# Gated attention and two FFNs on one core: the last two blocks of the first FFN in groups of 15 block products

## The reference

```python
# attention: 4 x 8 heads, 768 steps, head size 48; f = sigmoid(f_logit)
for t in range(S):
    state = f[:, :, t, :, None] * state + np.einsum('bhd,bhe->bhde', k[:, :, t], v[:, :, t])
    y[:, :, t] = np.einsum('bhd,bhde->bhe', q[:, :, t], state)
# x: 3072 tokens x 384
x = ((x @ w_a) * (x @ w_b)) @ w_out            # first FFN, 1536 hidden
p = domain_probs / (domain_probs.sum(-1, keepdims=True) + 1e-09)
for e in range(4):                             # second FFN, 4 x 1024 hidden
    h = np.maximum(x @ w1[e], 0.0)
    out += p[:, e:e + 1] * (h @ w2[e])
```

## Time and profile before

| | us |
|---|---|
| median of 3 runs | 1306.95 (1306.39 to 1307.71) |
| the profiled execution | 1305.98 |
| its span, first to last instruction | 1304.2 |
| PE busy | 1297.3 (99%) |
| DVE busy | 847.8 (65%) |
| ACT busy | 621.1 (48%) |
| POOL busy | 548.4 (42%) |

### The profile page before, as it was taken

How to read it: one execution, slowest core, us unless ns; L and a number is a source line. 1 busy time by engine, 2 the same in 40 slices (tenths; PEclk the granted TensorE clock), 3 DMA queues, 4 the chain that set the end, 5 groups by cost and what they waited for, 6 DMA issues and landing times.

```text
span 1304.2 us, 25769 instructions
## 1 busy us (share of the span) xinstructions
PE 1297.3 (99%) x9391; PEld 1269.5 (97%) x9391; DVE 847.8 (65%) x1668; ACT 621.1 (48%) x1259; POOL 548.4 (42%) x560
## 2 busy tenths in 40 slices
PE   9999999999999999999999999999999999999998
PEld 8999999999999999999999999999999999999998
DVE  8866565566533324277777777777677776777765
ACT  7654444444332323355445554445544545545442
POOL 3331211222136764324445644446544447444441
PEclk9999999999999999999999999999999999999999
DMA  8512122122204343123222343222342323343211
GB/s 262 166 43 68 47 63 67 49 61 67 57 16 132 101 143 120 50 79 97 91 86 80 91 134 89 95 82 69 108 133 88 98 64 95 96 130 98 88 59 49
DMA packets 71695, 117.74 MB, mean 90 GB/s; under 512 B 7120, under 2 KB 49808, under 8 KB 71568
## 3 DMA queue, kind: packets, MB, share of 16 engines
q1 hardware_dynamic: 71568, 116.08, 29.4%
HBM read 102.94 MB, written 14.55 MB: 90 GB/s over the span
## 4 chain that ended last, share of the span: by engine, by line
PE 98%; DVE 1%; DMA 0%; POOL 0%; issue 0%; ACT 0%; SPq 0%; DVEq 0%; POOLq 0%
PE bank L1964 12%; PE bank L1966 11%; PE bank L1965 11%; PE bank L2198 11%; PE bank L2199 10%; PE bank L2200 10%; PE bank L2094 5%; PE bank L2092 5%; PE bank L2093 5%; PE score_banks L2092 3%; PE score_banks L2094 3%; PE score_banks L2093 3%; PE bank L1954 2%; PE bank L1958 2%; PE score_banks L1883 1%; PE score_banks L1912 1%
## 5 line engine op out<-in xcount | busy, mean ns | idle before, releaser
L1291 POOL TENSOR_TENSOR wu<-w_r,wu 128x640 fp32r<-128x640 f32 (+1 forms) x132 | 200.6, 1522 | 314.8 <-ACT wu L976 314.8
L2198 PE MATMUL bank<-wd,h_hi 128*128 128x384 f32 x768 | 259.9, 338 | 0.3 <-issue 0.3
L2199 PE MATMUL bank<-wd,h_hi 128*128 128x384 f32 x768 | 257.6, 335 | 0.0
L2200 PE MATMUL bank<-wd,h_lo 128*128 128x384 f32 x768 | 257.1, 335 | 0.0
L1733 DVE SCALAR_TENSOR_TENSOR xt<-bank,pn,xt 128x384 f32<-128x384 f32 x288 | 177.1, 615 | 100.5 <-PE bank L2200 91.2
L1003 ACT ACTIVATE h_hi<-h 128x384 fp32r<-128x384 f32 x240 | 124.6, 523 | 192.9 <-DVE h L1683 81.1
L1964 PE MATMUL bank<-xs_hi,wab 128*128 128x384 f32 x570 | 196.7, 345 | 0.4 <-ACT a_sb L1014 0.4
L1965 PE MATMUL bank<-xs_hi,wab 128*128 128x384 f32 x570 | 191.0, 335 | 0.0
L1966 PE MATMUL bank<-xs_lo,wab 128*128 128x384 f32 x570 | 190.9, 335 | 0.0
L1296 POOL TENSOR_TENSOR wd<-raw,wd 128x384 fp32r<-128x384 f32 x128 | 133.4, 1056 | 87.6 <-ACT wd L981 83.6
L1704 DVE SCALAR_TENSOR_TENSOR h_lo<-h,h_hi 128x384 fp32r<-128x384 f32 x240 | 135.6, 579 | 50.1 <-ACT h_hi L1003 45.0
(11 more groups left out here) (203 smaller groups left out, 2668.1 us busy)
## 6 DMA issues: line engine op xcount, KB each, us to landing
w_r<-weight_sums SPq DMA_DIRECT2D x120, 320.0 KB, 2.9
raw<-w SPq DMA_DIRECT2D x48, 576.0 KB, 3.9
unit<-fkq SPq DMA_DIRECT2D x28, 504.0 KB, 4.5
v_in<-v_chunks SPq DMA_DIRECT2D x32, 144.0 KB, 4.1
out<-xt SPq DMA_DIRECT2D x24, 192.0 KB, 4.4
weight_sums<-w_s SPq DMA_DIRECT2D x10, 384.0 KB, 4.5
weight_sums<-w SPq DMA_DIRECT2D x40, 64.0 KB, 2.8
raw<-w SPq DMA_DIRECT2D x6, 384.0 KB, 3.2
```

Of the source, the lines that this page charges most:

```text
L1291: eng.tensor_tensor(wu_piece(g, n, 1), wu_raw(g, n), wu_piece(g, n, 0).bitcast(f32), ALU.subtract).then_inc(s_ulo, 1)
L2198: eng.matmul(o, hh, w_hi, start=(f == fs[0]), stop=False)
L2199: eng.matmul(o, hh, w_lo, start=False, stop=False)
L2200: mm = eng.matmul(o, hl, w_hi, start=False, stop=(f == fs[-1]))
```

## The change

Only 6 blocks of the first FFN run in the plain way (`PLAIN` = 6, `N1` = 72 hidden tiles). The last two blocks become a pass of groups of 15 products like those of the second FFN. `PASSES` lists one pass of the first FFN and four of the second, `GROUPS` all of their groups. The pass has 8 groups of three hidden tiles each, alternately for a (`makes_a`, into `h2`) and for b (`makes_h`, into `hb`). POOL multiplies the two (`product`, 6 operations per pair of groups), ACT rounds (`h1_round`), DVE makes the rest (`h1_rest`), and PE applies the down weights for a pair of groups in the next two groups (`down`), with DVE adding the tiles (`weigh`).

```diff
+    PLAIN = 6
+    N1 = PLAIN * FT1
+    PASSES = [(1, b) for b in range(PLAIN // 2, NP)] + [(2, b) for b in range(NP)]
+    GROUPS = [(p, q) for p, (ffn, _) in enumerate(PASSES) for q in (range(2 * NF) if ffn == 1 else (NQ, *range(NQ)))]
+    NS = 2 * NF + NQ
...
-    SUMS_AT, SUMS_PACE = CMIN_AT, 8
+    SUMS_AT, SUMS_PACE = 31, 9
```

```diff
                 if n == 0:
                     eng.wait_ge(s_wr, w_loads(q))
-                    eng.wait_ge(s_wst[q % 2], W_STORED * (q // 2)) if q >= 2 else eng.wait_ge(s_y, NU)
+                    if q:
+                        sums_stored(eng, q - 1)
...
+            def product(g, n):
+                o = H_ORDER[n]
+                eng.wait_ge(s_add, adds(g) + (3, 6, 7, 8, 9, 10)[n])
+                eng.tensor_tensor(hb[:, o, :], h2[:, o, :], hb[:, o, :], ALU.mult).then_inc(s_mul, 1)
```

The running sum of a unit was one scan of 384 elements, with a buffer of factors that reset it, and a minimum; it becomes six scans of 64:

```diff
-                if u >= FIRST:
-                    c = unit_ring[ring(u)][0:P2, F, :]
-                    eng.tensor_tensor_scan(c, reset[0:P2, :], c, 0.0, ALU.mult, ALU.add).then_inc(s_scan, 1)
-                    eng.wait_ge(s_scan, u - FIRST + 1)
-                    eng.tensor_scalar(c, c, CMAX, None, ALU.min).then_inc(s_cum, 1)
-                    return
-                for cc in range(CPU):
-                    c = unit_ring[ring(u)][0:P2, F, cc * CH:(cc + 1) * CH]
-                    eng.tensor_tensor_scan(c, c, cmax[0:P2, :], 0.0, ALU.add, ALU.min).then_inc(s_cum, 1)
+                n = CH if u < FIRST else HC
+                for cc in range(UT // n):
+                    c = unit_ring[ring(u)][0:P2, F, cc * n:(cc + 1) * n]
+                    eng.tensor_tensor_scan(c, c, cmax[0:P2, 0:n], 0.0, ALU.add, ALU.min).then_inc(s_cum, 1)
```

Operations of DVE on two tensors in SBUF become `scalar_tensor_tensor` with a factor of 1; those that read PSUM (`gate`, `add`) stay:

```diff
+            def two_inputs(to, a, b, op):
+                return eng.scalar_tensor_tensor(out=to, in0=a, scalar=1.0, in1=b, op0=ALU.mult, op1=op)
...
-                eng.tensor_tensor(h_lo[:, i % 2, 0:TB1], h_sb[:, :], h_hi[:, i % 2, 0:TB1].bitcast(f32),
+                two_inputs(h_lo[:, i % 2, 0:TB1], h_sb[:, :], h_hi[:, i % 2, 0:TB1].bitcast(f32),
                                   ALU.subtract).then_inc(s_hlo, 1)
```

On PE the down tiles of the first FFN stand in other places than those of the second:

```diff
+                    elif ffn(g) == 2:
+                        down(g - 1, n)
+                    elif makes_a(g):
+                        if n == 2:
+                            down(g - 1, 0)
+                        elif n == 5:
+                            down(g - 1, 1)
+                    elif q_of(g) > 1:
+                        if n == 0:
+                            down(g - 2, 2)
+                        elif n == 3:
+                            down(g - 2, 3)
+                        elif n == 5:
+                            down(g - 2, 4)
+                            down(g - 2, 5)
```

More of the change, by code:

```diff
@@ L356, in gated_attention_then_two_ffns @@
         s_wcp = sem("s_wcp")
[L357 removed]
+        s_wst = sem("s_wst")
         s_wu = [sem(f"s_wu{n}") for n in range(3)]
@@ L508, in f_tiles, with makes_a, makes_h, full @@
+        def makes_a(g):
+            return ffn(g) == 1 and q_of(g) % 2 == 0
+        def makes_h(g):
+            return not makes_a(g)
+        def full(g):
+            return ffn(g) == 1 or q_of(g) < NQ
+        def sums_of(g):
+            return q_of(g) if ffn(g) == 1 else 2 * NF + q_of(g)
         def f_tiles(q):
             return range(FG * q, FG * q + (FG if q < NQ else LAST))
-        def shares(g):
-            fs = f_tiles(g % GP)
+        def fs_of(g):
+            return range(FG) if ffn(g) == 1 else range(len(f_tiles(q_of(g))))
@@ L526, in results, with products, parts @@
+        def products(g):
+            return sum(2 * FG if ffn(x) == 1 and makes_h(x) else 0 for x in range(g))
         def results(g):
-            return sum(2 * len(f_tiles(x % GP)) for x in range(g))
+            return sum(2 * len(fs_of(x)) for x in range(g) if makes_h(x))
+        def parts(g):
+            return len(shares(q_of(g))) if ffn(g) == 2 else 1
         def tiles(g):
-            return sum(TT * len(shares(x)) for x in range(g))
+            return sum(TT * parts(x) for x in range(g) if makes_h(x))
@@ L1079, in _ @@
                     split_hi(HI_AT[j])
-                for n in range(1, NB1):
+                for n in range(1, PLAIN):
                     for k in range(KT):
@@ L1101, in _ @@
                     copy(g, 0)
                     copy(g, 1)
-                    if g:
-                        up_round(g + 1, 0)
-                    if change:
-                        x2_round(change, 0)
-                        x2_round(change, 1)
+                    for n in range(FG):
+                        down_round(g, n)
+                    plain_hi(nxt, 2)
+                    for n in range(3):
+                        sum_hi(nxt, n)
+                    copy(g, 2)
+                    plain_hi(nxt, 3)
@@ L1108, in _ @@
+                    up_round(g + 2, 0)
+                    h2_round(g, 4)
+                    up_round(g + 2, 1)
+                    h2_round(g, 5)
+                    up_round(g + 2, 2)
+                    down_round(g + 1, 0)
+                elif full(g):
+                    copy(g, 0)
+                    copy(g, 1)
+                    for n in range(FG):
+                        down_round(g, n)
                     copy(g, 2)
                     h2_round(g, 0)
-                    if g:
-                        up_round(g + 1, 1)
@@ L1318, in _ @@
                             x1_lo(n, k)
-                for q in range(NQ):
+                for q in range(NS):
                     for n in range(16):
```

810 lines of the change are left out of this document (517 added, 293 removed).

## The result

The changed kernel takes 1413.4 us (median of 4 runs, 1408.3 to 1418.4), the kernel before 1307.1 (1306.4 to 1307.7): a ratio of 1.081 with a 95% interval of 1.080 to 1.083. The prediction had 1301.3 us and faster: sign and size are wrong. The profiled execution took 1408.3, its span is 1406.5 us.

What follows compares the result with a forecast made beforehand. It took PE, busy 99% of the span, as the bound. 1305.98 - 12.5 + 0.7 + 0.2 + 3.2 + 1.3 + 1.5 = 1300.4, with the runs' median 0.97 higher: 1301.3 us, range 1296.5 to 1308.

Steps and rivals of the forecast that it cites:

- every rival: Full gain 1294 to 1298, 0.16; attention 1305 to 1309, 0.17; POOL's sums 1312, 0.08; POOL with DVE 1312, 0.05.
- 72 matmuls less, 12.5 us: First FFN's last two blocks: four pairs of groups save 72 matmuls at 0.1738 us each, 12.5 us less.
- The scalar costs 0: DVE's operations on two SBUF tensors: `scalar_tensor_tensor` takes as long as `tensor_tensor`, 0 with 2 ns each way.
- a budget: Pair of groups in the new pass: POOL 19.1, DVE 17.9 and ACT 12.7 us, none reaching PE's 25.0.
- a pass above 183 us: Sign of being wrong: a pass of the second FFN takes more than 732 / 4 = 183 us.
- POOL and DVE together, the last rival: New pass: from 2.3 us more blocking a pair they pass PE's 25.0; at 5 us, 1312; chance 0.05.
- Groups 0 to 2, 1.25 + 0.25 + 1.0 + 1.2: New pass's start: PE waits before products 4 and 13 of group 1, then products 2 and 4 of group 2.
- the -0.5: Change of stage at the new pass's start: the 0.56 us that PE idles there goes, -0.5.
- Groups 4 and 6, 0.3 each: New pass, groups for a: PE waits 0.3 us before product 4 for `copy` 0 and `add` 1, +0.7 in all.
- Groups 3 and 5, 0.2: New pass, groups 3 and 5: `add` 6 is ready 0.5 us early; +0.2 for meetings of DVE with POOL.
- The last group, 1.3: New pass's last group: `add` 7 ends at 11.6 where product 14 is due at 10.4, +1.3 us.
- The attention, 1.5: Attention beside weight sums: a down product waits 0.2 us for a late rest in 7 of 22 units, +1.5.
- The last groups of the second FFN's passes, 0: Last groups of second-FFN passes, 17 us long: `add` 7 is over 1 us early, so 0.

Runs made afterwards that it cites:

- e1: The changed kernel with only the operations on two SBUF tensors as plain `tensor_tensor` again; 1416.3 us.
- e4: The changed kernel with ACT's order in groups 1 to 8 of second-FFN passes as in the kernel before, which spreads POOL's rests; 1331.7 us.
- e5: e4 with the first FFN pass's input sums moved from the ends of groups for a to behind `add` 4 and 6; 1326.1 us.
- e7: e4 with first-FFN-pass input sums behind adds 7, 8, 10, POOL's rests later, some between products, and ACT's last group reordered as in e6; 1323.2 us.
- e9: e7 with rests of down weights right behind those of wu again and input sums behind adds 8, 9 and 10; 1318.1 us.
- e6: e4 with ACT, in the first FFN pass's last group, rounding the last two products before the next down weights' first piece; 1330.9 us.
- e10: e9 with the last four of POOL's eleven input-sum rests moved from second-FFN passes' last groups to the following group of two hidden tiles; 1314.5 us.
- e8: The kernel before with only ACT's rounding order changed in second-FFN groups, so POOL's six rests run as one stretch; 1375.4 us.
- e3: The changed kernel with POOL beginning its rests of wu only after product 4 in the second FFN's full groups; 1341.3 us.

## Why the prediction was wrong, by its steps

The measured 1413.4 us lies far outside the range, 1296.5 to 1308, and above every rival, of which the dearest was 1312. What the single terms became, by the account above (what PE loses, in us):

- **72 matmuls less, 12.5 us**: right. The page has 72 fewer, the spacing is 0.174 us.
- **The scalar costs 0**: right, shown by e1.
- **The second FFN's groups**: the step that failed. The prediction has no term for them, and only "0" for the last groups of the passes; they cost 74.5 + 22.1 - 4.1 = 92.5. It saw that ACT rounds three pieces of weights for group 2 at the end of group 0, priced that at +1.25 there, and did not ask in which other groups ACT's list reads like that: 35 in the second FFN. The only argument that it has for groups is a budget, POOL's 19.1 us and DVE's share of 25.0 in a pair of the first FFN, and in the second FFN a budget shows nothing: POOL is busy 49% of a pass of the changed kernel, 52% in e4 and 51% in the kernel before; DVE 78, 76 and 74%, with its stretched operations counted in. What changed is that the work lies in one stretch, in the 7 us ahead of `add` 1. From the changed kernel to e4 that is 65 us of waits and 18 of lower clock in the second FFN. The prediction did name a pass above 183 us as a sign of being wrong, and it came; only its 183 is a quarter of a stretch that holds less than four passes, and a pass of the kernel before takes 186.1.
- **POOL and DVE together, the last rival**: the right mechanism, at a chance of 0.05 and with the wrong price. It counted 0.45 us of DVE's work for each of eight operations as a share of a pair's 25.0 us, and asked for a full pair; what an operation waits was in its own row, 1.25 us where 0.56 is usual, and it did not add that up along DVE's queue. Each operation of DVE on two SBUF tensors took 1.3 to 1.9 us in the stretch, 0.8 to 1.35 more than alone, and four in a row with `add` 1 behind them need no full engine.
  The Trainium skill, "SBUF — State Buffer", section "SBUF: two separate sides", says that the one that starts first holds the port pair for its whole instruction; the trace agrees: each of the four ended 0.41 to 0.42 us after one of POOL's instructions, and `add`s, with one input in PSUM, did not wait.
- **Groups 0 to 2, 1.25 + 0.25 + 1.0 + 1.2**: 1.20, 0.27, 1.23 and 1.90. The chain was read rightly, the sum was 0.9 too small, nearly all of it in the last. The idle time at the same change of stage did go, as the -0.5 said.
- **Groups 4 and 6, 0.3 each** (0.6 in all, the sum has 0.7): 1.9 each, since the last rests of a pair stand beside POOL's first rests of the next. **Groups 3 and 5, 0.2**: 0.2 and 2.0, the latter by input sums beside POOL. **The last group, 1.3**: 1.5 at `add` 7, but 2.9 at its product 4 and 1.8 behind it as well. The waits before product 4 are the same omission as in the second FFN; e5 shows it for group 5 and the last group, e7 and e9 for groups 4 and 6 and for the place of POOL's work. The wait at `add` 7 stayed in every run, at 0.5 to 2.0, and was not taken further.
- **The attention, 1.5** (the 0.2 in 7 units that it names make 1.4): PE waited 0.3 us for `h_lo` in all, and the 4000th matmul stood at 368.63 against 368.20, so 0.4. That mark moves by up to 1.8 us between traces, 1.5 of it in the first 60 us; from the 500th matmul to the 4000th the cost is 0.4 to 0.8 in ten of the eleven traces of the changed kernel and its edits, 1.5 in e6. The sums of weights beside the units were nearly free.
- **The last groups of the second FFN's passes, 0**: 3.1 in each of three passes, in four waits. e10 shows POOL's eleven rests as the cause of a part; the two waits that stayed were not taken further.
- **The clock**: no term at all. In the second FFN it fell only behind waits of PE, so it is no loss of its own, but it adds a quarter to theirs.

Open: why waits of the same place come in two sizes (gaps of 2.0 and 3.4 us before product 4 of group 4, in e6 and e4, whose code there is the same). That a rest of DVE misses one of POOL's instructions or two would explain it; it was only argued.

## What to carry to other kernels

When a scheduler's list is reordered for one stage, look for every stage that shares the lines, and ask of each engine that follows not how much it does but when. GpSimd's work in one stretch across a point where DVE has several two-input SBUF operations ahead of a result that PE waits for costs each of them the rest of a GpSimd instruction, here 0.8 to 1.35 us; spread over the group, the same work left PE no such wait. Budgets of busy time don't see this. And once PE waits, count the clock too: here another 21.8 us beside 90.9 of waits.

## What the runs showed of the hardware

- **Clock after a wait.** Behind eight of the nine waits of 3.5 us in the changed kernel's trace, 10 to 17 matmuls started 0.32 us apart, 384 columns at 1.2 GHz where 2.4 is 0.17; behind the other it was 7 such matmuls. Behind waits of 2.0 us and three of 2.75 it was none, behind one of 2.2 us ten. In e8, four of the nine waits of 3.5 us were followed by no such matmul and the other five by 9 to 11, two of three waits of 2.75 by 9; in e4, 16 of them stood behind four waits of 0.4 to 2.1 us within 13 us, at a granted clock of 0.50. So the length of a wait alone does not decide it. In all it cost a quarter of what the waits themselves did, 21.8 to 90.9 us. The Trainium skill, "TensorE: Matmul & The Clock Gate", section "Part 1: The HAM clock gate (the "warmup" mystery)", names the half clock as the state of an idle array; the traces agree in so far as it came only behind waits.
- **Some orders scatter more from run to run.** The kernel before lies within 0.1% over the four runs beside the changed one (0.2% over nine later ones), the changed one within 0.7% (1408.3 to 1418.4), e6 within 0.6%, but e3 within 0.1% and e7 within 0.06%. Why is not shown.
- **POOL is slowed too, by little:** its rests of `wu` take 1786 ns in the mean from 560 us on, 1597 before.
